# Fifteen slots with two units in place of twelve, and batch 1's combinations two to four slots earlier, in a fused attention and MLP kernel

## What is computed

```
scores = scale * q @ k.T                    # 4 batches, 8 heads, 576 x 576, head_dim 64
kth = 32nd largest score of each row
attn = softmax(where(scores >= kth, scores, -1e9)) @ v
x = attn, heads side by side                # 4 x 576 x 512
mixed = real(fft(fft(x, axis=1), axis=2)); u = x + mixed
x = u + relu(norm(u) @ w_ch1) @ w_ch2       # first MLP, 512 -> 2048 -> 512
out = x + relu((norm(x) * g_ln) @ w1) @ w2  # second MLP
```

## Time and profile before

| | |
|---|---|
| median of 3 runs | 1364.39 us (1364.19 to 6670.84) |
| profiled execution | 1364.6 us, its span 1362.8 us |
| TensorE matmul busy | 1245.7 us, 91% of the span |
| VectorE busy | 1112.6 us, 82% |
| ScalarE, GpSimd busy | 786.3 us, 350.7 us |
| chain that ended last | PE 57%, DVE 35%, issue 5% |

### The profile page before, as it was taken

How to read it: one execution, slowest core, us unless ns; L and a number is a source line. 1 busy time by engine, 2 the same in 40 slices (tenths; PEclk the granted TensorE clock), 3 DMA queues, 4 the chain that set the end, 5 groups by cost and what they waited for, 6 DMA issues and landing times.

```text
span 1362.8 us, 22760 instructions
## 1 busy us (share of the span) xinstructions
PE 1245.7 (91%) x7944; PEld 1019.1 (75%) x7944; DVE 1112.6 (82%) x2224; ACT 786.3 (58%) x1564; POOL 350.7 (26%) x308
## 2 busy tenths in 40 slices
PE   5776778999999699799998999999999999999999
PEld 3444444787777578688886888888689999999997
DVE  7999999899999997999899889976585454646453
ACT  4777765577776556576675557653444444444442
POOL 2444430122122242132344222322121121222210
PEclk9989988999999999999999999999999999999999
DMA  7999993566767647787795577763254343333342
GB/s 249 320 339 340 330 321 146 191 222 222 243 192 256 199 159 242 243 277 252 235 314 198 170 249 235 259 212 110 77 170 139 124 147 124 124 124 124 124 147 85
DMA packets 117395, 280.63 MB, mean 206 GB/s; under 512 B 29729, under 2 KB 29730, under 8 KB 117282
## 3 DMA queue, kind: packets, MB, share of 16 engines
q1 hardware_dynamic: 105522, 231.98, 51.5%
q10 hardware_dynamic: 10368, 42.47, 8.3%
q0 software_dynamic: 1392, 4.73, 1.0%
HBM read 235.87 MB, written 42.73 MB: 204 GB/s over the span
## 4 chain that ended last, share of the span: by engine, by line
PE 57%; DVE 35%; issue 5%; POOL 1%; ACT 1%; DMA 1%; SPq 0%; DVEq 0%; ACTq 0%; POOLq 0%
PE Big L735 23%; PE Big L718 15%; DVE top L1110 15%; DVE wk L1116 14%; PE Sp L718 7%; DVE ex L1123 3%; PE Tp L667 3%; PE Tp L689 2%; PE Sp L762 2%; PE Sp L774 1%; DVE st L1202 1%; PE Tp L794 1%; PE Big L762 1%; DMA sc<-sc_ahead 0%; PE Big L774 0%
## 5 line engine op out<-in xcount | busy, mean ns | idle before, releaser
L735 PE MATMUL Big<-wr,hh 128*128 128x512 f32 x1152 | 361.9, 395 | 0.0
L718 PE MATMUL Big<-uh,wr 128*128 128x256 f32 (+1 forms) x1384 | 315.5, 318 | 6.2 <-ACT hh L964 5.7
L1110 DVE MAX8 top<-wk 128x8 f32<-128x576 f32 x432 | 304.4, 746 | 0.0
L718 PEld LDWEIGHTS Big<-uh,wr 128*128 128x128 f32 x1384 | 233.3, 191 | 26.2 <-issue 16.2
L735 PEld LDWEIGHTS Big<-wr,hh 128*128 128x128 f32 x1152 | 217.7, 189 | 41.3
L735 PE MATMUL Big<-wr,hl 128*128 128x512 f32 x576 | 239.1, 415 | 3.6 <-DVE wr L1255 2.6
L500 POOL TENSOR_TENSOR hl<-hf,hh 128x256 fp32r<-128x256 f32 (+1 forms) x123 | 107.5, 874 | 454.5 <-ACT hh L964 454.4
L718 PE MATMUL Big<-ul,wr 128*128 128x256 f32 (+1 forms) x692 | 215.3, 311 | 0.0
L1116 DVE MATCH_REPLACE8 wk<-top,wk 128x576 f32<-128x576 f32 x288 | 211.5, 742 | 0.0
L667 PE MATMUL Tp<-ident,ex 128*128 128x128 f32 x720 | 117.3, 289 | 55.7 <-DVE ex L1123 50.5
L910 ACT ACTIVATE pT<-Tp 128x640 f32<-128x640 f32 x144 | 101.1, 702 | 108.0 <-PE Tp L667 107.8
(11 more groups left out here) (133 smaller groups left out, 1787.9 us busy)
## 6 DMA issues: line engine op xcount, KB each, us to landing
wf<-in_weights SPq DMA_DIRECT2D x206, 512.0 KB, 3.5
wr<-w_low SPq DMA_DIRECT2D x246, 256.0 KB, 4.2
sc<-in_weights SPq DMA_DIRECT2D x50, 512.0 KB, 3.2
sc<-sc_ahead ACTq DMA_DIRECT2D x36, 576.0 KB, 5.3
w_low<-wr SPq DMA_DIRECT2D x32, 512.0 KB, 6.5
sc_ahead<-U ACTq DMA_DIRECT2D x18, 576.0 KB, 5.2
sc_ahead<-un ACTq DMA_DIRECT2D x9, 576.0 KB, 4.1
sc_ahead<-yb ACTq DMA_DIRECT2D x9, 576.0 KB, 6.5
```

The lines of the kernel that those rows point to most:

```text
L718: last = nc.tensor.matmul(hidden(n), a[:, kd * P:(kd + 1) * P], x[:, kd, 0:P * SIZE[p]], start=(kd == 0 and j == 0), stop=(kd == KD - 1 an ...
L735: last = nc.tensor.matmul(Ac[:, j, :], a[:, n % 2, j * P:(j + 1) * P], w, start=(f == 0 and m == 0), stop=(f == KF - 1 and m == 2))
L1110: nc.vector.max(top[:, s % RING, r, :], src).then_inc(s_top, 1)
```

## The change

```diff
-DOUBLE = (52, 66, 86, 90, 96, 101, 105, 111, 121, 126, 132, 138)
+DOUBLE = (45, 49, 53, 57, 62, 66, 70, 74, 82, 85, 104, 112, 121, 134, 139)
...
-    return {1: 78, 2: 116, 3: 148}[b] + i // 2
+    return {1: 76, 2: 116, 3: 148}[b] + i // 2
...
-    return NT * (b + 1) + 2 + ((0, 0, 1, 1, 2, 3)[i] if b == 1 else i)
+    return NT * (b + 1) + (1 + i // 2 if b == 1 else 2 + i)
...
-                        if n == NT // 2 * (b + 1) + 5 + b + j:
+                        if n == NT // 2 * (b + 1) + (4 + j // 2 if b == 1 else 7 + j):
```

## The result

The changed kernel takes 1372.38 us (median of 4 runs, 1371.59 to 1372.69) against 1364.29 us: 1.0065 of the time before, 95% interval 1.0053 to 1.0077, 8 us slower. The forecast was 1357 us, 7 us faster, with a range of 1346 to 1370. The profiled execution took 1372.4 us, its span 1370.5 us, where the forecast had 1355.6.

The account below looks back on a forecast made before the run. TensorE and VectorE were taken to bound the kernel by turns. Slot 142 3.8 us later, less 11.0 us gained at the end, gave -7.2: a span of 1355.6 us, about 1357 us in time, range 1346 to 1370.

Parts of the forecast that it names:

- A narrow unit 2.9 us, slots 60 and 72: Slots 40 to 71: a narrow unit costs TensorE 2.9 us; slot 60 starts at 390.0, slot 72 at 458.5.
- Gone is the stall of group 3's transposes, but TensorE was waiting for VectorE there anyway: Slots 72 to 75: 4.01 us transpose stall goes, though TensorE waited for VectorE anyway; slot 76 at 484 (before 480.9).
- I charge 2 us: Slot 76: batch 1's folds end near 488, piece 0 would be reached at 486, so 2 us is charged.
- rival (e): TensorE's clock: new idle at slots 82 and 84 could cost 1 to 3 us, 1360 us; forecast with it 0.42.
- I keep that cost as it is: Masks beside GpSimd: 1.82 us instead of 0.82, 1.0 us more, kept since GpSimd's steps move only among pairs.
- Two waits ahead of L1187: Batch 1's combinations: VectorE stands 3.4 and 2.6 us; pair 45 starts at 572.6 (before 565.3).
- Rival (b): Same place, pieces later: gain gone if slot 76 starts at about 492, 1373 us at 500; chance 0.22.
- (a): From slot 76: folds in time, `sums(1)` does not wait, VectorE regains 5 to 8 us; 1350 us; 0.30 with (c).
- (c): Ahead of slot 144: this part takes no longer than before; 1352 us; chance 0.30 together with (a).
- (d): Slots 40 to 141: all 37.0 us of TensorE idle fill up, 1327 us; 0.03 including more than half of it.
- Slots 102 to 115, 12 us of idle: VectorE sets this stretch's end, slot 116 at 738.1 (before 736.7), and TensorE idles 12 us in it.
- The tail, 11.0 us gained: Behind slot 144: three wide units leave, 12.5 us, less 1.5 us charged for slots 144 to 147: 11.0 us gained.

Follow-up runs that it names:

- Experiment 7: Changed kernel with group 2's residual and store moved behind batch 1's folds on GpSimd; 1368.07 us, ratio 1.0039.
- experiment 4: Kernel before with batch 1's chain moved as in the change, keeping its own twelve double slots; 1371.32 us, ratio 1.0061.
- experiment 2: Changed kernel with all three combinations of batch 1 behind pair 41; 1369.87 us, ratio 1.0049.
- experiment 10: Experiment 9's kernel with group 6's gains ahead of batch 2's pairs and folds on GpSimd; 1355.14 us, ratio 0.9938.
- experiment 12: Changed kernel, combinations unmoved, with only the GpSimd edits of experiments 7, 9 and 10; 1359.55 us, ratio 0.9973.
- Experiment 9: Changed kernel with the edits of experiments 2 and 7, plus group 7's residual behind batch 3's fold; 1360.71 us, ratio 0.9972.
- experiment 11: Kernel before with fifteen double slots, old chain, and the GpSimd edits of experiments 9 and 10; 1363.53 us, ratio 1.0007.
- experiment 1: Changed kernel with the double slot 74 moved to 81; 1374.9 us, ratio 1.0080.

## Why the prediction was wrong

**A narrow unit 2.9 us, slots 60 and 72**: right. Slots 40 to 59 took 114.2 us (forecast 115.3), slot 72 started at 458.6 (458.5). One piece of that is right by luck: there is no wait ahead of L1132. VectorE came to it at 458.23, not at 455: it had stood 2.3 us up to 409.0 for ScalarE's copy of the scores (L869) and 3.0 us once for GpSimd's 1/std, and had longer masks. Pair 37's start, 460.8, is as forecast only because this happens to be the time, 458.2, that the forecast had for the end of TensorE's slot 71.

**"Gone is the stall of group 3's transposes, but TensorE was waiting for VectorE there anyway", slot 76 at 484**: the step that failed. The stall was taken from L535 and given to L500. I listed what now stands on GpSimd, costed it against the folds ("I charge 2 us"), and did not ask for the low half of the slot's second unit, queued in the same place and needed sooner than the folds. Behind that wait the same matmuls also ran at half clock for 5.3 us, 2.6 us that the forecast had only in rival (e). Experiment 7 puts the residual away: slot 76 starts at 485.8 and slot 78 at 506.7. This is worth 3.5 us of time alone.

**"I keep that cost as it is"** for masks beside GpSimd: mis-sized. GpSimd's steps met the masks of pairs 36 to 38 and cost 1.4 to 1.6 us in each pair; pair 38 ends 2.8 us later than forecast. The Trainium skill (SBUF — State Buffer, Who interferes with whom) says that a VectorE instruction with two SBUF inputs contends with a GpSimd instruction that reads SBUF, and that one with a single SBUF input, outside the modes that use both ports, does not. These traces agree: a mask of 0.8 us took up to 2.25 beside GpSimd's normalising steps of 1.9 us (3.77 for two), a fold of 0.42 us took 1.49 beside additions of 1.5 us (4.40 for three), while MAX8 and MATCH_REPLACE8 beside the same steps kept their 0.75 us. The forecast weighed this rule only for combinations, and charged it nothing.

**Two waits ahead of L1187, "the shortened chain makes VectorE 7 us later, not earlier"**: right in kind, and the two waits in size: 2.66 and 3.59 us were measured (3.4 and 2.6 forecast). Pair 45 began 12.6 us later than before, 5.3 us more than forecast; experiment 4 shows 6.2 for the chain alone. What the forecast missed is that this needn't be paid: experiment 2 puts the combinations a pair later and takes 2.2 us off by the ratios, and for the same edit experiment 10 stands 4.8 us below experiment 12.

**Rival (b)** is what happened, at the place named, with slot 76 at 491.7 where 492 was named as the point at which the gain is gone. It had the cause wrong (dearer units; a GpSimd queue in truth), and its scale of a microsecond for each microsecond held: +7.7 at slot 76, +7.7 at slot 102, +9.5 at slot 142. By that alone the span would be 1365.1. (a), (c) and (d) did not occur. (e), the clock, is 0.86 in slots 72 to 75 against 0.89 before and 0.96 in slots 76 to 82 against 0.97: a part of the loss there, not its bulk. Behind slot 142, where the forecast looked for no clock loss, it is the larger part: 3.5 of 5.4 us.

**Slots 102 to 115, 12 us of idle**: 14.7 measured, of which 4.5 are the two waits for the gains. Those were to be found by the same reading as in batch 1: group 6 starts four slots earlier, batch 2's steps keep their slots, so they meet. Experiment 10 takes 3.1 us off.

**The tail, 11.0 us gained**: 5.6 measured, the second term that failed. The charge of 1.5 us was for VectorE's work in slots 144 to 147; what GpSimd does there was not asked. Group 7's residual lengthened batch 3's folds, TensorE waited 2.51 us for them, and a stretch at half clock followed. Experiment 9 sets it right at 11.3 us gained (447.3 less 436.0), so the forecast's term itself is right once the residual is out of the way.

So the sum was that of a kernel whose GpSimd stands in nobody's way. Experiment 12 is that kernel: a span of 1357.6 us against the forecast's 1355.6. What stays open: why the stretch at half clock behind a wait is so different in length, and how much of a difference of 2 to 3 us between two medians is chance, since executions of one kernel here lie up to 5.5 us apart (experiment 11) and the number of long ones among them varies. Experiments 12 and 10 are such a case: 4.8 us apart by the ratios, and 1.6 at slot 142 of their traces. Slots 76 to 82 take 60.8 us in the one and 56.8 in the other, the same 4 us as in experiment 2, but the trace of experiment 10 has 2.0 us more in slots 72 to 75 (29.4 against 27.4), in instructions that are the same in both.

## What to carry to other kernels

Moving a stage on an in-order engine means asking of every instruction now queued behind it who needs it and when, not only of the stage's own results: here a low half of 0.7 us behind 8.8 us of other work. When a table shifts all later stages by three slots, look at each place where a stage that moved meets one that did not. Here group 7's residual at batch 3's fold cost 5.8 us and group 6's gains behind batch 2's pairs 3.1, where the whole change aimed at 7. And a change that loses can be sound: it was 0.6% slower as written, 0.3% faster with GpSimd's queue put right, and 0.6% faster with the combinations a pair later as well. Fifteen doubles (another table) with the old chain, and GpSimd's queue put right at batches 2 and 3, gave nothing that can be measured. The shortened chain with twelve doubles and GpSimd's queue put right was not run, so how much of the gain needs the doubles isn't known.

## What the runs showed of the hardware

A stall of TensorE can cost more than its length, since the work right behind it can run at half clock, and how long it does so varied much. Behind 3.99 us of waiting in the changed kernel it was 5.3 us; its Fourier pieces came 6 us behind the wait and took the full-clock 2.38 us. Behind 3.33 us in experiment 1's kernel it was 13.1 us, and two pieces took 4.46 and 4.29 us. Behind 2.51 us ahead of batch 3's first piece, the clock was 0.73 over 12.8 us; without this wait and with the folds in time, 5.8 us were gone, of which only 2.1 were the wait. Behind a wait of 2.08 us (at 472.9 in the changed kernel) the matmuls ran at the full clock. Identical instructions differ too: slots 74 and 75 of experiments 9 and 10 had clocks of 1.00 and 0.89. What sets the length these runs do not settle.

GpSimd's additions and VectorE's instructions with two SBUF inputs hinder each other in both directions. The residual's two additions took 3.00 us beside a mask and 2.50 alone; the masks' excess over 0.8 us is about 14.3 us over the changed kernel from pair 20 on, against 8.3 before.
